# Own tile for M6+M1, tokens one pair ahead, late part splits, double raw weights, and a DVE swap in each pair of a fused channel-attention and FFN kernel

## The chip, the cores and the metric

The kernel runs on one core of one Trainium2 chip. The metric is device time in microseconds (us). The kernel before took 1188.86 us, the median of 3 runs (1186.72 to 1191.2). The profiled execution took 1185.15 us, of which its span, from the first to the last instruction, is 1183.3 us.

## What is computed

Channel attention over two batches of 6016 tokens and 256 channels, and on its result a feed-forward block with 2048 hidden units:

```python
qn = q / (norm(q, axis=1) + 1e-6);  kn = k / (norm(k, axis=1) + 1e-6)
s = softmax(kn.transpose(0, 2, 1) @ qn / tau)      # 256 x 256 per batch
x = (v @ s).reshape(12032, 256)
h = x @ w_in                                       # 256 -> 2048
g = h * (1 / (1 + exp(-h)))
out = g @ w_out                                    # 2048 -> 256
```

## The kernel before, in words

**Attention, 0 to about 98 us.** q and k stream in, TensorE sums the scores, DVE and ACT make norms and softmax. The softmax is folded into w_in (`fold`), so that v is never multiplied by it: each batch gets its own first weights. For the second batch they are saved to DRAM (`a1_dram`) and loaded again pair by pair (`load_a1`, `prepare_a1`, `split_a1`).

**Feed-forward, 98 us to the end.** 12 steps of tokens (`it` 0 to 11); a step holds two column halves of 512 tokens, steps 5 and 11 of 448. Each step runs over 8 pairs of hidden blocks; `n` = 8 * `it` + `pair` counts them through, 0 to 95. Both matrix products use a seven-product (Strassen-Winograd) scheme on 2x2 blocks; every product is three matmuls, since each operand is split into a rounded part and the rest (hi and lo): hi*hi, hi*lo, lo*hi. A pair from n = 9 on is 14 products, 42 matmuls: p1 to p7 of the first product (`product`, L802 to L804), and f22, f11, f21, f_t1 to f_t4 of the second (`second`, L860 to L862). Step 0 uses plain products for the second part (`output`, L847 to L851), 45 matmuls a pair.

**The engines' parts in a pair.** ACT copies the first product's sums out of PSUM (`seed_u1`, L1143, is its first on a new pair, then `copy_u`, `silu_c11`, `copy_w`), applies silu, rounds (`round_h`, `round_t13`, `round_t4`, `round_t2`) and flushes the product f21 to `fl` (`flush`). DVE makes C22 and C21 (`make_c22`, L1532, for which p4 waits; `make_c21`), the sums t1 to t4, and every "lo" part (`split_h`, L1546, and others). Each engine runs its list in order; nothing is reordered.

**Outputs.** The products M1, M3 to M7 gather in PSUM over the 8 pairs of a step. In the next step they are copied out: pair 0 `copy_m3`, `copy_m1` (to `o1`); pair 1 `copy_m7`, `copy_m4`, `copy_m5`; pair 2 `sum_u` on DVE (L1606) adds M6 to `o1` **in place**; pair 3 `make_nv`; pair 4 `sum_c22`. The output blocks are summed in DRAM by accumulating DMAs that POOL issues in order: `add_flushed` once a pair (`fl`, L627/L629), `add_o7` and `add_o1` in pair 1 (L640, L634), `add_u` in pair 2, `add_nv` in pair 3. `flush` of a pair waits until the `fl` store of the pair before has landed. `sum_u` writes the tile that `add_o1` reads, so it waits for that DMA's landing:

```python
dve.wait_ge(used_t2, PAIRS * it)
dve.wait_ge(o1_stored, 16 * it)
nc.vector.tensor_tensor(o1[:, 0:tok], m6[:, 0:tok], o1[:, 0:tok], ALU.add).then_inc(u_summed, 1)
```

`add_o7` stands ahead of `add_o1` on POOL and waits for `begin_c21`, an SP store that waits for `copy_m4` in pair 1.

**Tokens.** For the step to come, SP loads six blocks (`load_x`, in pair 7 before `load_ring_b`), POOL adds five more onto them by accumulating DMAs (`add_x_first`, three, in pair 2; `add_x_second` in pair 3; `add_x_third` in pair 6, after the split of T2), ACT rounds seven blocks in pairs 2 to 7 (`ROUND_X`) and DVE splits them in pairs 3 to 7 (`SPLIT_X`), T3 and T4 in the pair that rounds them.

**Second weights.** w_out's combinations for the later steps (8 parts) are made in steps 0 and 1: `load_part` on SP, `part` on POOL, `split_part` on DVE, `store_part` on SP; they come back each pair as `ring` (`load_ring_a`, 640 KB; `load_ring_b`, 256 KB).

## Time and profile before

| | before |
|---|---|
| median of 3 runs | 1188.86 us |
| profiled execution / its span | 1185.15 / 1183.3 us |
| TensorE busy with matmuls | 1065.1 us, 90% |
| DVE busy | 930.7 us, 79% |
| ACT busy | 912.0 us, 77% |
| POOL busy | 293.5 us, 25% |
| DMA queue of POOL (software) / of SP | 24.2% / 38.9% of 16 engines' span |
| mean granted TensorE clock | 0.963 |

Busy time of TensorE counts pipelined matmuls, so 90% doesn't mean that it runs at its peak 90% of the time. No engine is near 100%; what sets the time is read stage by stage from the waits and the timeline.

### The profile page before, as it was taken

The numbers are of one execution on the slowest core, as the hardware profiler recorded it, in microseconds if no ns is written. First come the engines' busy times: TensorE is split into PE (matmuls) and PEld (weight loads), VectorE is DVE, ScalarE is ACT, GpSimd is POOL, SyncE is SP. The second block draws the span as 40 slices with busy tenths as digits, with TensorE's granted clock in tenths as the row PEclk, the third lists the DMA queues.
The fourth block names the chain that finished last, engine by engine and source line by source line (L and its number), as shares of the span: only waits on it lengthen the run. The fifth ranks groups of instructions, "written<-read, shape, count | busy, mean of one in ns | idle before, by whom it ended". The sixth has DMA issues, their size and how long they took to land.

```text
span 1183.3 us, 15134 instructions
## 1 busy us (share of the span) xinstructions
PE 1065.1 (90%) x4584; PEld 862.6 (73%) x4584; DVE 930.7 (79%) x1306; ACT 912.0 (77%) x1581; POOL 293.5 (25%) x321
## 2 busy tenths in 40 slices
PE   9999899799899899899698898899799899899897
PEld 7987677577677677687587676687687687687786
DVE  6887665698698698698598898788688688688697
ACT  7988566687788788788577786788787788788775
POOL 3790430231211211211544351120211211211100
PEclk9999899999899899899899999999999999999899
DMA  9960722676676766666585774775675675674642
...
DMA packets 107841, 197.06 MB, mean 167 GB/s; under 512 B 9424, under 2 KB 42320, under 8 KB 107632
## 3 DMA queue, kind: packets, MB, share of 16 engines
q1 hardware_dynamic: 82720, 150.07, 38.9%
q0 software_dynamic: 24608, 45.39, 24.2%
...
q10 hardware_dynamic: 432, 0.62, 0.1%
...
## 4 chain that ended last, share of the span: by engine, by line
PE 50%; ACT 15%; DMA 13%; DVE 10%; issue 8%; SPq 1%; POOL 1%; DVEq 0%; ACTq 0%; POOLq 0%
PE ps_h L802 9%; DMA out_t_dram<-o_sb 8%; PE ps_h L803 8%; PE ps_h L804 8%; PE ps_o L860 5%; PE ps_o L861 5%; PE ps_o L862 5%; PE ps_h L860 3%; PE ps_h L862 3%; PE ps_h L861 3%; ACT ps_h L1043 3%; ACT gx_hi L1203 2%; ACT h L1159 2%; DVE g_lo L1546 2%; ACT w L1151 2%
## 5 line engine op out<-in xcount | busy, mean ns | idle before, releaser
L1546 DVE TENSOR_TENSOR g_lo<-h,g_hi 128x512 fp32r<-128x512 f32 (+1 forms) x296 | 204.0, 692 | 39.2 <-ACT g_hi L1182 36.6
L802 PE MATMUL ps_h<-b_hi,a_hi_mid 128*128 128x512 f32 (+1 forms) x336 | 141.4, 421 | 60.2 <-ACT h L1159 53.2
L627 POOL DMA_DIRECT2D out_t_dram<-fl_sb x70 | 60.6, 866 | 532.2 <-ACT fl_sb L1210 525.5
L1182 ACT ACTIVATE g_hi<-h 128x512 fp32r<-128x512 f32 (+1 forms) x296 | 182.5, 620 | 10.5 <-PE ps_h L862 3.8
L803 PE MATMUL ps_h<-b_lo,a_hi_mid 128*128 128x512 f32 (+1 forms) x336 | 136.0, 405 | 0.0
L804 PE MATMUL ps_h<-b_hi,a_lo_mid 128*128 128x512 f32 (+1 forms) x336 | 135.3, 403 | 0.0
L802 PEld LDWEIGHTS ps_h<-b_hi,a_hi_mid 128*128 128x128 f32 x336 | 67.1, 200 | 90.5 <-ACT h L1159 58.9
L860 PE MATMUL ps_h<-g_hi,ring 128*128 128x512 f32 (+1 forms) x264 | 103.6, 393 | 13.3 <-DVE h L1541 6.1
L1580 DVE TENSOR_TENSOR gx_lo<-t_raw,gx_hi 128x1024 fp32r<-128x1024 f32 (+1 forms) x88 | 107.0, 1216 | 1.0 <-ACT gx_hi L1189 0.9
L1558 DVE TENSOR_TENSOR t_raw<-h 128x1024 f32<-128x1024 f32 (+1 forms) x88 | 105.3, 1196 | 0.0
L860 PE MATMUL ps_o<-gx_hi,ring 128*128 128x512 f32 (+1 forms) x264 | 102.7, 389 | 0.7 <-DVE gx_lo L1590 0.4
L862 PE MATMUL ps_h<-g_hi,ring 128*128 128x512 f32 (+1 forms) x264 | 102.9, 390 | 0.0
L861 PE MATMUL ps_h<-g_lo,ring 128*128 128x512 f32 (+1 forms) x264 | 102.7, 389 | 0.0
L861 PE MATMUL ps_o<-gx_lo,ring 128*128 128x512 f32 (+1 forms) x264 | 102.4, 388 | 0.0
L862 PE MATMUL ps_o<-gx_hi,ring 128*128 128x512 f32 (+1 forms) x264 | 102.4, 388 | 0.0
L1203 ACT ACTIVATE gx_hi<-h 128x512 fp32r<-128x512 f32 (+1 forms) x88 | 54.3, 617 | 58.5 <-DVE h L1575 58.2
L1585 DVE TENSOR_TENSOR g_lo<-t_raw,g_hi 128x512 fp32r<-128x512 f32 (+1 forms) x88 | 60.8, 690 | 41.7 <-ACT g_hi L1197 41.2
L1189 ACT ACTIVATE gx_hi<-t_raw 128x1024 fp32r<-128x1024 f32 (+1 forms) x88 | 90.5, 1028 | 0.8 <-PE ps_o L862 0.7
L1210 ACT ACTIVATE fl_sb<-ps_h 128x512 f32<-128x512 f32 (+1 forms) x81 | 48.0, 593 | 54.9 <-PE ps_h L862 53.7
L1172 ACT ACTIVATE h<-h 128x512 f32<-128x512 f32 (+1 forms) x96 | 59.5, 620 | 38.6 <-DVE h L1532 38.0
L802 PE MATMUL ps_h<-b_hi,a_hi_last 128*128 128x512 f32 (+1 forms) x168 | 67.4, 401 | 23.4 <-DVE h L1532 23.4
L1541 DVE TENSOR_TENSOR h<-ps_h,u 128x512 f32<-128x512 f32 (+1 forms) x96 | 65.1, 678 | 22.4 <-PE ps_h L804 21.8
...
## 6 DMA issues: line engine op xcount, KB each, us to landing
ring<-s_dram SPq DMA_DIRECT2D x88, 640.0 KB, 4.9
ring<-s_dram SPq DMA_DIRECT2D x88, 256.0 KB, 3.2
out_t_dram<-fl_sb POOLq DMA_DIRECT2D x72, 256.0 KB, 5.8
x_raw<-v_t_dram SPq DMA_DIRECT2D x58, 256.0 KB, 4.0
x_raw<-v_t_dram POOLq DMA_DIRECT2D x45, 256.0 KB, 6.5
out_t_dram<-o_sb POOLq DMA_DIRECT2D x36, 256.0 KB, 5.2
out_t_dram<-o_sb SPq DMA_DIRECT2D x27, 256.0 KB, 2.7
...
```

The lines of the kernel that those rows point to most:

```text
L802: nc.tensor.matmul(out, w_hi, x_hi, start=start, stop=False, skip_group_check=True)
L803: nc.tensor.matmul(out, w_hi, x_lo, start=False, stop=False, skip_group_check=True)
L804: return nc.tensor.matmul(out, w_lo, x_hi, start=False, stop=True, skip_group_check=True)
L860: nc.tensor.matmul(out[:, 0:tok], w_hi, x_hi[:, 0:tok], start=start, stop=False, skip_group_check=True)
L861: nc.tensor.matmul(out[:, 0:tok], w_hi, x_lo[:, 0:tok], start=False, stop=False, skip_group_check=True)
L862: return nc.tensor.matmul(out[:, 0:tok], w_lo, x_hi[:, 0:tok], start=False, stop=True, skip_group_check=True)
L1182: nc.scalar.activation(g_hi[:, g, 0:tok], h[:, g, 0:tok], ACT.Copy).then_inc(hi[g], 1)
L1189: nc.scalar.activation(gx_hi[:, GT1:GT3 + 1, 0:tok], t13_raw[:, :, 0:tok], ACT.Copy).then_inc(t13_hi, 1)
L1203: nc.scalar.activation(gx_hi[:, GT4, 0:tok], h[:, H21, 0:tok], ACT.Copy).then_inc(t4_hi, 1)
L1546: nc.vector.tensor_tensor(g_lo[:, g, 0:tok], h[:, g, 0:tok], g_hi[:, g, 0:tok].bitcast(F32), ALU.subtract).then_inc(lo[g], 1)
L1558: nc.vector.tensor_tensor(t13_raw[:, :, 0:tok], h[:, H11:H12 + 1, 0:tok], h[:, H12:H22 + 1, 0:tok], ALU.add).then_inc(t13_made, 1)
L1580: nc.vector.tensor_tensor(gx_lo[:, GT1:GT3 + 1, 0:tok], t13_raw[:, :, 0:tok], gx_hi[:, GT1:GT3 + 1, 0:tok].bitcast(F32), ALU.subtract).the ...
```

## The change

- `sum_u` writes a tile of its own, `u_sum`; its wait for `add_o1`'s landing becomes one for the copy of M1, and for the output work of the step before. `copy_m1` now waits for the landing of `add_o1` of the step before.
- Tokens: `add_x_first`, `add_x_second`, `add_x_third` go from pairs 2, 3, 6 to 0, 1, 5 (from step 2 on; for step 2's tokens the old places stay). ACT's roundings are reordered, one pair ahead of DVE's splits. TensorE's p4 alone waits for the last group. `load_x` goes behind `load_ring_b` and `load_a1`.
- Raw second-batch weights and their sums get two tiles each, with new places of the reload.
- DVE: `make_c22` goes ahead of `split_h(H11)` in each pair. In step 0 the part and token splits go to the end of a pair, one part a pair from pair 1; `split_part` of the turning pair (n = 8) goes to its end; `sum_c22` from pair 4 to 5.
- POOL rounds three quarters of w_out instead of ACT; SP's `load_x(1)` goes ahead of the wait for the folds; ACT loads the silu table early; the last C12 store goes from POOL to ACT.

```diff
+        u_sum = sb("u_sum_sb", [P, TOK])
+        a1_raw1 = sb("a1_raw1", [P, 4, P])
+        sums1 = sb("sums1", [P, 4, P])
...
-        reload_at = {SWITCH + max(2 * pair - 1, 0): pair for pair in range(PAIRS)}
+        reload_at = {SWITCH + 1 + 3 * pair // 2 + pair // 6: pair for pair in range(PAIRS)}
...
             def load_a1(pair):
                 sp.wait_ge(a_split, PAIRS)
-                if pair:
-                    sp.wait_ge(a1_split, pair)
-                sp.dma_start(a1_raw[:], a1_dram[:, pair]).then_inc(a1_loaded, 16)
+                if pair >= 2:
+                    sp.wait_ge(a1_split, pair - 1)
+                sp.dma_start(a1_raw[pair % 2][:], a1_dram[:, pair]).then_inc(a1_loaded[pair % 2], 16)
...
+            sp.wait_ge(v_split, 3)
+            load_x(1)
             sp.wait_ge(wp_summed, 2 * FOLDS)
             load_part(0)
             load_part(1)
-            sp.wait_ge(v_split, 3)
-            load_x(1)
...
-                if pair == PAIRS - 1 and it + 2 < ALL:
-                    sp.wait_ge(x_split, 3 + FACTORS * it)
-                    load_x(it + 2)
                 load_ring_b(n)
                 if n + 1 in reload_at:
                     load_a1(reload_at[n + 1])
+                if pair == PAIRS - 1 and it + 2 < ALL:
+                    sp.wait_ge(x_split, x_groups(it + 1))
+                    load_x(it + 2)
...
+            for n in range(1, PARTS):
+                round_wo(n)
             add_x_first(1)
             part(0)
...
-                if pair == 2 and it + 1 < ALL:
+                if pair == (0 if it > 1 else 2) and it + 1 < ALL:
                     add_x_first(it + 1)
-                if pair == 3 and it + 1 < ALL:
+                if pair == (1 if it > 1 else 3) and it + 1 < ALL:
                     add_x_second(it + 1)
-                if pair == 6 and it + 1 < ALL:
+                if pair == (5 if it > 1 else 6) and it + 1 < ALL:
                     add_x_third(it + 1)
...
                 if it > 1:
-                    act.wait_ge(c21_stored, 32 * (it - 1))
+                    act.wait_ge(o1_stored, 16 * (it - 1))
+                    act.wait_ge(u_summed, it - 1)
                 nc.scalar.activation(o1[:, 0:tok], m1[:, 0:tok], ACT.Copy).then_inc(o1_copied, 1)
...
-            ROUND_X = {2: (B11, B21), 3: (B22,), 4: (T2,), 5: (T1,), 6: (T3,), 7: (T4,)}
+            ROUND_X_SECOND = {2: (B11, B21), 3: (B22,), 4: (T2, T1), 5: (T3,), 7: (T4,)}
+            ROUND_X = {2: (B11, B21), 3: (T2, B22), 4: (T1,), 5: (T3,), 6: (T4,)}
...
-            SPLIT_X_FIRST = {4: (T1, T3), 5: (B11, B22), 7: (T4, T4)}
-            SPLIT_X = {3: (B11,), 4: (B21,), 5: (B22, T2), 6: (T1, T3), 7: (T4,)}
+            SPLIT_X_FIRST = {3: (T1, T2), 4: (T3, T3), 6: (B11, B22), 7: (T4, T4)}
+            SPLIT_X_SECOND = {3: (B11, B21), 4: (B22,), 5: (T2, T1), 6: (T3,)}
+            SPLIT_X = {3: (B11,), 4: (B21, T2), 5: (B22,), 6: (T1, T3), 7: (T4,)}
...
                 dve.wait_ge(used_t2, PAIRS * it)
-                dve.wait_ge(o1_stored, 16 * it)
-                nc.vector.tensor_tensor(o1[:, 0:tok], m6[:, 0:tok], o1[:, 0:tok], ALU.add).then_inc(u_summed, 1)
+                dve.wait_ge(o1_copied, it)
+                if it > 1:
+                    dve.wait_ge(c21_stored, 32 * (it - 1))
+                    dve.wait_ge(nv_made, it - 1)
+                nc.vector.tensor_tensor(u_sum[:, 0:tok], m6[:, 0:tok], o1[:, 0:tok], ALU.add).then_inc(u_summed, 1)
...
-            PARTS_AT = {2: (0, 1), 3: (2,), 4: (3,), 6: (4,), 8: (5,), 10: (6,), 12: (7,)}
+            PARTS_AT = {1: 0, 2: 1, 3: 2, 4: 3, 6: 4, 8: 5, 10: 6, 12: 7}
...
+                if PAIRS - EARLY - 1 <= n < PAIRS - 1:
+                    split_a(0, n + 1)
+                if n < PAIRS - 2:
+                    sum_a(0, n + 2)
+                if n in PARTS_AT:
+                    split_part(PARTS_AT[n])
                 if n in SPLIT_X_FIRST:
                     split_x(1, *SPLIT_X_FIRST[n])
...
+                make_c22(n, tok)
                 split_h(n, tok, H11)
-                make_c22(n, tok)
                 split_t2(n - 1, before)
```

## Rows read from the trace of the kernel before

**Rows 1.** Waits, whole run: who waited for whom: us in total, times, longest

```profile
DVE o_sb L1606 <- DMA out_t_dram<-o_sb: 58.9, 10, 10.1
PEld ps_h L802 <- DVE h L1532: 47.1, 49, 2.2
DVE b_lo L1507 <- ACT b_hi L1129: 22.4, 20, 1.5
```

**Rows 2.** Timeline, ACT's L1143 at seven pair starts: start us, us, instruction

```profile
117.48 0.60 ACT L1143 ACTIVATE ps_h<-ps_h 128x512 f32<-128x512 f32 x1
201.68 0.58 ACT L1143 ACTIVATE ps_h<-ps_h 128x512 f32<-128x512 f32 x1
292.76 0.59 ACT L1143 ACTIVATE ps_h<-ps_h 128x512 f32<-128x512 f32 x1
302.37 0.59 ACT L1143 ACTIVATE ps_h<-ps_h 128x512 f32<-128x512 f32 x1
...
557.34 0.54 ACT L1143 ACTIVATE ps_h<-ps_h 128x448 f32<-128x448 f32 x1
741.07 0.59 ACT L1143 ACTIVATE ps_h<-ps_h 128x512 f32<-128x512 f32 x1
1093.05 0.54 ACT L1143 ACTIVATE ps_h<-ps_h 128x448 f32<-128x448 f32 x1
```

**Rows 3.** Timeline, step 2, pair 2; in brackets idle before and releaser

```profile
310.68 1.22 POOL L634 DMA_DIRECT2D out_t_dram<-o_sb  x1
311.98 0.57 POOL L629 DMA_DIRECT2D out_t_dram<-fl_sb  x1
319.01 0.69 DVE L1606 TENSOR_TENSOR o_sb<-ps_o,o_sb 128x512 f32<-128x512 f32 x1 [6.08 <-DMA out_t_dram<-o_sb]
321.50 0.79 PE L802 MATMUL ps_h<-b_hi,a_hi_mid 128*128 128x512 f32 x1 [5.70 <-ACT h L1159]
```

**Rows 4.** Windows: stretch, length; busy (instructions) by engine; granted clock, DMA share, GB/s

```profile
322.00:325.00 3.00, 3.00 (x8) 2.31 (x7) 1.42 (x3) 2.11 (x5) 1.53 (x2) 0.51 1.02 155
347.40:357.50 10.10, 9.89 (x44) 7.80 (x43) 9.31 (x14) 8.72 (x15) 0.87 (x1) 1.00 0.48 117
357.50:368.50 11.00, 9.83 (x43) 7.77 (x42) 9.34 (x14) 8.72 (x15) 1.76 (x2) 1.00 0.62 135
```

**Rows 5.** Timeline, step 2, pair 6, around C22

```profile
363.72 0.69 DVE L1507 TENSOR_TENSOR b_lo<-x_raw,b_hi 128x512 fp32r<-128x512 f32 x1 [0.86 <-ACT b_hi L1129]
...
365.67 0.50 PE L802 MATMUL ps_h<-b_hi,a_hi_last 128*128 128x512 f32 x1 [1.17 <-DVE h L1532]
```

**Rows 6.** DMA issues, 309 to 322 us: KB each, us to landing

```profile
ring<-s_dram SPq DMA_DIRECT2D x1, 640.0 KB, 9.2
out_t_dram<-fl_sb POOLq DMA_DIRECT2D x1, 256.0 KB, 8.1
```

**Rows 7.** Timeline, steps 5 and 6, the reload: ring wait, output wait, preparation's ends

```profile
580.35 0.47 PE L860 MATMUL ps_h<-g_hi,ring 128*128 128x448 f32 x1 [4.21 <-DMA ring<-s_dram]
587.66 0.69 DVE L1606 TENSOR_TENSOR o_sb<-ps_o,o_sb 128x512 f32<-128x512 f32 x1 [10.11 <-DMA out_t_dram<-o_sb]
...
601.12 2.12 POOL L664 TENSOR_TENSOR sums<-a_raw 128x128 f32<-128x128 f32 x1
607.38 1.01 POOL L675 CAST a_hi_mid<-sums 128x512 fp32r<-128x512 f32 x1
```

**Rows 8.** Timeline, step 0: the tokens of step 1, and TensorE's longest stop

```profile
125.83 2.80 POOL L582 DMA_DIRECT2D x_raw<-v_t_dram  x3 [35.83 <-DMA x_raw<-v_t_dram]
...
142.64 0.79 PE L847 MATMUL ps_o<-g_hi,wo_hi 128*128 128x512 f32 x1 [4.78 <-DVE g_lo L1546]
```

**Rows 9.** Timeline, attention: a POOL cast alone, a DVE sum beside a POOL instruction

```profile
45.43 1.04 POOL L535 CAST w_in_hi<-w_in_raw 128x1024 fp32r<-128x1024 f32 x1
...
84.95 2.82 DVE L1433 TENSOR_TENSOR square_sum<-square_sum 128x512 f32<-128x512 f32 x1
```

**Rows 10.** Timeline, step 1, pair 2: ACT waits for the tokens

```profile
232.68 1.15 ACT L1129 ACTIVATE b_hi<-x_raw 128x512 fp32r<-128x512 f32 x2 [6.45 <-DMA x_raw<-v_t_dram]
```

More of the change, by code:

```diff
@@ L277, in channel_attention_ffn @@
         used_t4 = sem("used_t4")
-        part_loaded = sem("part_loaded")
+        part_loaded = [sem(f"part_loaded{n}") for n in range(2)]
         part_step = sem("part_step")
@@ L285, in channel_attention_ffn @@
         a1_saved = sem("a1_saved")
-        a1_loaded = sem("a1_loaded")
+        a1_loaded = [sem(f"a1_loaded{n}") for n in range(2)]
         a1_step = sem("a1_step")
@@ L345, in width, with x_groups, x_place @@
             return tokens_of(n // PAIRS)[1]
-        reload_at = {SWITCH + max(2 * pair - 1, 0): pair for pair in range(PAIRS)}
+        reload_at = {SWITCH + 1 + 3 * pair // 2 + pair // 6: pair for pair in range(PAIRS)}
+        assert all(SWITCH + pair < n <= SWITCH + PAIRS - 2 + pair for n, pair in reload_at.items())
+        X_FIRST = ((T1, T2), (T3, T3), (B11, B22), (T4, T4))
+        X_SECOND = (B11, B21, B22, T2, T1, T3, T4)
+        X_LATER = (B11, B21, T2, B22, T1, T3, T4)
+        def x_groups(step):
+            return len(X_FIRST) + FACTORS * (step - 1)
+        def x_place(step, block_):
+            if step == 1:
+                return 1 + [block_ in range(a, b + 1) for a, b in X_FIRST].index(True)
+            return x_groups(step - 1) + 1 + (X_SECOND if step == 2 else X_LATER).index(block_)
         def part_tiles(i):
@@ L493, in _ @@
                     begin_c21(it - 1)
-                if it > 1 and pair == 4:
+                if it > 1 and pair == 5:
                     store_c22(it - 1)
-                if pair == PAIRS - 1 and it + 2 < ALL:
-                    sp.wait_ge(x_split, 3 + FACTORS * it)
-                    load_x(it + 2)
                 load_ring_b(n)
@@ L596, in add_x_third @@
             def add_x_third(step):
-                if step == 1:
-                    pool.wait_ge(x_split, 1)
-                else:
-                    pool.wait_ge(x_split, 3 + FACTORS * (step - 2) + 4)
+                pool.wait_ge(x_split, x_place(step, T2))
                 add_x(step, X_T2, 1, 0).then_inc(t_third, 16)
@@ L655, in prepare_a1 @@
             def prepare_a1(pair):
-                a12, a22, a11, a21 = (a1_raw[:, j, :] for j in range(4))
-                s1, s2, s3, s4 = (sums[:, j, :] for j in range(4))
-                pool.wait_ge(a1_loaded, 16 * (pair + 1))
-                if pair:
-                    pool.wait_ge(a1_split, pair)
+                raw, totals = a1_raw[pair % 2], a1_sums[pair % 2]
+                a12, a22, a11, a21 = (raw[:, j, :] for j in range(4))
+                s1, s2, s3, s4 = (totals[:, j, :] for j in range(4))
+                pool.wait_ge(a1_loaded[pair % 2], 16 * (pair // 2 + 1))
+                if pair >= 2:
+                    pool.wait_ge(a1_split, pair - 1)
                 else:
@@ L673, in prepare_a1 @@
                 pool.wait_ge(p4_done, SWITCH + pair + 1)
-                nc.gpsimd.tensor_copy(a_hi(pair)[:, 0:3, :], a1_raw[:, 0:3, :])
-                nc.gpsimd.tensor_copy(a_hi(pair)[:, 3:7, :], sums[:]).then_inc(a1_rounded, 1)
+                nc.gpsimd.tensor_copy(a_hi(pair)[:, 0:3, :], raw[:, 0:3, :])
+                nc.gpsimd.tensor_copy(a_hi(pair)[:, 3:7, :], totals[:]).then_inc(a1_rounded, 1)
             split_rows(0)
@@ L834, in p4 @@
                 pe.wait_ge(c22_made, n + 1)
+                if pair == 0 and n:
+                    pe.wait_ge(x_split, x_groups(n // PAIRS))
                 product(pair, par, tok, BANK_Y, A22, T4, False).then_inc(p4_done, 1)
@@ L1259, in opening_pair @@
                 seed_u1(0, TOK)
-                round_wo(1)
+                nc.scalar.activation(scratch[:, 0:1], ones[:, 0:1], ACT.Silu)
                 copy_folded(1, 0)
@@ L1296, in first_step @@
                 copy_w(n, TOK)
+                if n >= 3 and n - 3 < len(X_FIRST):
+                    round_x(1, *X_FIRST[n - 3])
                 silu_c22(n, TOK)
@@ L1344, in pair_step @@
                 if it < FINAL:
-                    for block_ in ROUND_X.get(pair, ()):
+                    for block_ in (ROUND_X if it > 1 else ROUND_X_SECOND).get(pair, ()):
                         round_x(it + 1, block_, block_)
@@ L1667, in pair_step @@
                     make_nv(it - 1)
-                if it > 1 and pair == 4:
+                if it > 1 and pair == 5:
                     sum_c22(it - 1)
@@ L1673, in pair_step @@
                 if it < FINAL:
-                    for block_ in SPLIT_X.get(pair, ()):
+                    for block_ in (SPLIT_X if it > 1 else SPLIT_X_SECOND).get(pair, ()):
                         split_x(it + 1, block_, block_)
+                make_c22(n, tok)
                 split_h(n, tok, H11)
-                make_c22(n, tok)
                 split_t2(n - 1, before)
                 make_c21(n, tok)
-                for i in PARTS_AT.get(n, ()):
-                    split_part(i)
+                if it == 1 and pair == PAIRS - 1:
+                    split_x(2, T4, T4)
+                if n in PARTS_AT:
+                    split_part(PARTS_AT[n])
                 if n - 1 in reload_at:
```

89 lines of the change are left out of this document (42 added, 47 removed).

## The prediction, made before the changed kernel was run

> **What bounds the kernel now.** I read four views in this order. First the waits of the whole run, to see which long waits are on an engine that the others need. DVE waits ten times, once for each output step, 58.9 us in all, for a DMA to land before `sum_u` [rows 1]; TensorE waits 49 times for C22, and DVE 20 times for a rounded token block [rows 1]. POOL's far longer waits don't count: POOL is idle three quarters of the time. Second the starts of the pairs, by ACT's first copy of a pair. The pair from 292.76 to 302.37 us took 9.61 us [rows 2] for its 42 matmuls, 0.229 us each: that is TensorE without a stop, the floor of a wide pair, and 8 of them make 76.9 us. But steps 2 to 4 took 557.34 - 292.76 = 264.6 us and steps 7 to 10 took 1093.05 - 741.07 = 352.0 us [rows 2]: seven wide steps, 616.6 us, 88.1 each. So 11.2 us of each step is lost. Third the timeline of one step, to see where. In pair 2 DVE stands 6.08 us before `sum_u`, everything behind it in DVE's list stands too, and TensorE stands 5.70 us [rows 3]. After that the granted clock is 0.51, the 1.2 GHz level, and 8 matmuls take 3.00 us [rows 4], which is 0.375 us each or more; some 9 matmuls at about 0.2 us too much are 1.8 us. In pairs 6 and 7 DVE waits 0.86 us for ACT's rounding, then splits the block, then H11, and only then makes C22; TensorE stands 1.17 us, and the granted clock stays 1.00 (2.4 GHz) [rows 4, 5]. Two of those with their restart are 2.8 us. 5.7 + 1.8 + 2.8 = 10.3 of the 11.2; the other 0.9 us are C22 waits of 0.1 to 0.4 us in the pairs between. Fourth the DMA views, for what comes next (below).
>
> **The wait for `add_o1` goes.** `sum_u` keeps its place, but its last wait is now a copy of pair 0. Its other new waits are on output work of the step before, over 60 us old. Nobody else waits for the landing until `copy_m1` of the next step, 80 us later. The addition costs DVE 0.69 us [rows 3], as `make_nv` does in pair 3, which has no stop of its own. Gain 5.7 + 1.8 = 7.5 us a step. The gain of the clock rests on there being no other long stop: the 1.17 us ones don't lower it [rows 4, 5].
>
> **C22 ahead of H11, roundings a pair ahead.** C22 needs p7 and `copy_w`, which are done when the second token split ends in a pair with two. Without the 0.86 us wait and without the 0.6 us of H11 in front of it [rows 5], C22 comes 1.4 to 1.5 us earlier, which is more than 1.17 us. H11's lo part is wanted only in the next pair. In pairs without a token block C22 now waits for p7 with H11 behind it, and C21 behind both; but C21 needs p4, nine matmuls (2.1 us) after p7, and C22, H11 and T2, some 0.6 us from start to start, take 1.9 us of that. Close, but it fits. Gain 2.8 + most of 0.9, I take 3.2 us a step (bounds 2.4 and 3.7).
>
> **What is late next: POOL's DMA queue.** `flush` of pair 3 needs the landing of pair 2's `fl` store. That store is issued right behind `add_o1`, at 311.98, and takes 8.1 us [rows 3, 6]: it lands at 320.1. With no stop, pair 3 begins 9.61 us after pair 2 and ACT wants the landing at about 320.7; only 0.6 us are left, and there is no slack between flush, seed and p6. The ring's 640 KB, issued at the same time, took 9.2 us [rows 6] and are wanted at about 322. The change puts `add_x_second` in front of that store. Its price: pair 6 has one accumulate of this kind more than pair 5, and the DMA engines' busy time is 0.62 x 11.0 = 6.8 against 0.48 x 10.1 = 4.8 us [rows 4], so 2.0 us if nothing overlaps, and nothing if it does. A few microseconds later in this pair the DMA engines are fully busy (share 1.02) [rows 4]. I take 1.4 us later, so a stop of 0.8 us in each step; bounds 0 and 3 (the whole 2.0 and a crowded pair 1: three `add_x_first`, 6 us of engine time, now fall in pair 0 beside the six loads). The three were behind `add_u` in pair 2 before and leave it. Wide step after: 76.9 + 0.5 (left-over C22 waits) + 0.8 = 78.2; seven steps 547.4; **gain 69.2 us** (bounds 77 and 50).
>
> **Reload, steps 5 and 6.** They took 741.07 - 557.34 = 183.7 us [rows 2] where the pairs' floors are 8 x 8.6 (448 tokens) + 76.9 = 145.7. With one raw tile, `load_a1` waits for the split of the pair before, and SP's ring load and `begin_c21` stand behind it: TensorE waits 4.21 us for the ring, DVE 10.11 us for `add_o1` [rows 7]. Two tiles take that away. What stays: each of 8 `split_a1` adds about 1.15 us to a DVE list that is busy 9.3 us in a pair with two token splits [rows 4], about 0.8 us over the floor, 6 us in all. New: `prepare_a1` takes POOL 7.3 us beside a busy DVE, from 601.12 to 608.39 [rows 7]. It now stands in pairs 1 and 2 of step 5, between the output DMAs and the `fl` store. The store of pair 2 then goes out about 9 us into the pair instead of 1, lands some 3 us after `flush` wants it, and the next is again about 2 us late: 5 us. Together with 5 us of DVE slowed beside POOL (it was so before): 145.7 + 16.3 = 162.0, **gain 21.7 us** (bounds 28 and 12).
>
> **Step 11** has the `sum_u` wait, no token blocks: **gain 7 us**.
>
> **Step 0.** POOL waits for the token loads at 125.83, then makes the parts; DVE's part splits wait for them in pair 2, and TensorE stands 4.78 us behind DVE [rows 8], with the slow clock after. Now the tokens come while SP idles, the part splits stand at the end of a pair, where DVE otherwise waits about 3 us for p7. Pairs 1 to 7 took 201.68 - 117.48 = 84.2 us [rows 2]; the floor is 45 x 0.229 = 10.3 each. I take 10.5, plus 1.15 us each in front of pairs 6 and 7, where `split_a` (a_lo wanted by p1) now stands behind H12: 75.8, gain 8.4. Three w_out roundings leave ACT in pair 0; TensorE is nearly without a stop there: gain 1.0. They go to POOL, 1.04 us each [rows 9], 3.1 us from 90.0 on, beside the DVE chain of the second softmax, for which TensorE waits. A DVE sum took 2.82 us beside a POOL instruction, 0.7 alone [rows 9]; the chain's instructions there mostly read PSUM or one operand; bounds 0 and 2.1, I take 0.5. **Gain 8.9 us** (bounds 11 and 3).
>
> The Trainium skill (SBUF — State Buffer, Who interferes with whom) says that a DVE instruction with two SBUF inputs contends with a GpSimd instruction that reads SBUF, and that one with at most one such input does not. That speaks against this move only if POOL's casts reach the chain's one multiplication of two SBUF tiles, at 93.55 us; the 2.82 us row agrees with the rule, and by it the cost would be 0, or at most one cast, 1.04 us.
>
> **Step 1** took 292.76 - 201.68 = 91.1 us. Its 6.45 us wait for tokens [rows 10] is not touched: `load_x(2)` still stands on SP behind the store of part 5, and that part's split, now at the end of the turning pair, is 1.7 us later. C22 and the roundings give about 4.5 in pairs 4 to 7. **Gain 3 us** (bounds 6 and -2). The last store's move to ACT is off the last chain: 0.
>
> **Sum.** 69.2 + 21.7 + 7 + 8.9 + 3 = 109.8 us. 1185.15 - 109.8 = 1075.4 us for an execution like the profiled one; the median of the runs is 3.7 us above it, so **1079 us**.
>
> **Rivals.** *The queue takes the place of the wait.* For it: 0.6 us of slack, DMA engines fully busy for a time in this pair [rows 4]. Against it: `fl`'s store landed only 1.2 us behind `add_o1` (318.9 and 320.1), so DMAs in this queue overlap. If `add_x_second` costs its whole latency like `add_o1` did, 5 to 6 us, pair 3 stops 4.4 us, the clock falls again, 6.3 us instead of 0.8 in ten steps: 1079 + 55 = 1134 us. Chance 0.11. The Trainium skill (DMA: Bandwidth & Descriptors, Queues, rings and completion order) says that a completion count is written only behind every earlier write of the same DMA engine, across its queues. By that `fl` can't be told as landed before the token block in front of it; how much that is it doesn't say, and it would give a time between the two.
>
> *POOL's DMAs are served one by one and become the bound; the kernel is slower.* 17 a step (8 `fl`, 4 outputs, 5 tokens). At 5.2 us each in order a step would be 88 us as before, and above that every step is slower: at 5.5 us 93.5, some 5.4 more in ten steps, +54, less 12 from steps 0 and 1: about 1230 us. The overlap of 1.2 us speaks against it: it decides only if tokens and stores packed into pairs 0 and 1 lose that overlap. Chance 0.02.
>
> *The stop stays*, since `sum_u` is not what TensorE needs: only the other terms, 109.8 - 10 x 7.5 = 35: 1144 us. The 5.70 us on TensorE right behind the 6.08 on DVE speaks against it. Chance 0.02.
>
> *Better than forecast*: no queue stop, POOL out of the way in step 5: about 1060 and below. Chance 0.05.
>
> **How the numbers follow.** The forecast has 0.80. Its own bounds, added as if independent around 1079, give about 1062 to 1105; the range goes a little towards the queue rival: 1060 to 1112. A measurement of this kernel tells about 0.5%, 6 us, from no change. All cases but one are far beyond that on the fast side: faster 0.97, slower 0.02, within 0.5% 0.01.
>
> **What would show it.** No idle time of DVE before `sum_u`; the store of `u_sum` issued 3 us into pair 2 instead of 9; no granted clock near 0.5 in steps 2 to 4; no wait of `b_lo` for `b_hi`; 78 us from step to step; a wait of ACT's `flush` for the landing of `fl` at pair 3 of about 0.8 us, and of 2 to 3 us at pairs 3 and 4 of step 5. The forecast is wrong if `flush` or the ring waits over 3 us in the common steps, or if DVE, with 9.3 us of work in a pair of 9.6 [rows 4], is late for other reasons than DMAs: then TensorE waits for C21, T4 or H11 where nothing does today.

## The result, and the profile after

The changed kernel takes **1072.47 us** (median of 4 runs, 1070.89 to 1073.94) against 1188.24 us (4 runs, 1186.72 to 1191.2): a ratio of 0.9023, 95% interval 0.9000 to 0.9046. The forecast was 1079 us. The profiled execution took 1070.89 us, its span 1069.1 us.

The page after, busy times and two rows of the 40 slices:

```profile
PE 1034.2 (97%) x4584; PEld 851.6 (80%) x4584; DVE 934.1 (87%) x1307; ACT 898.7 (84%) x1580; POOL 297.6 (28%) x323
...
PE   9999998989999999999978999999999999999997
...
PEclk9999999999999999999999999999999999999999
```

TensorE is now busy 97% of the span, and none of the 40 slices has a mean granted clock under 0.9; shorter drops are left (last section). The waits of the whole run that answer to [rows 1] (who waited for whom: us in total, times, longest):

```profile
DVE h L1558 <- PE ps_h L825: 41.7, 46, 5.2
...
ACT fl_sb L1234 <- DMA out_t_dram<-fl_sb: 9.5, 9, 2.8
...
PEld ps_h L823 <- DVE h L1558: 5.8, 9, 1.6
```

DVE's 58.9 us of waiting for `add_o1` have no row any more, nor have its waits for a rounded token block. TensorE's weight loads waited 47.1 us in 49 waits for C22 and wait 5.8 us in 9; it is DVE that now waits for TensorE before it can make C22, 41.7 us in all. The starts of pairs after, answering to [rows 2] (timeline, ACT's first copy: steps 0, 1, 2, its second and third pair, steps 5, 7 and 11):

```profile
99.76 0.61 ACT L1167 ACTIVATE ps_h<-ps_h 128x512 f32<-128x512 f32 x1
195.41 0.58 ACT L1167 ACTIVATE ps_h<-ps_h 128x512 f32<-128x512 f32 x1
280.54 0.59 ACT L1167 ACTIVATE ps_h<-ps_h 128x512 f32<-128x512 f32 x1
290.18 0.59 ACT L1167 ACTIVATE ps_h<-ps_h 128x512 f32<-128x512 f32 x1
300.76 0.59 ACT L1167 ACTIVATE ps_h<-ps_h 128x512 f32<-128x512 f32 x1
...
512.38 0.54 ACT L1167 ACTIVATE ps_h<-ps_h 128x448 f32<-128x448 f32 x1
679.80 0.59 ACT L1167 ACTIVATE ps_h<-ps_h 128x512 f32<-128x512 f32 x1
987.93 0.54 ACT L1167 ACTIVATE ps_h<-ps_h 128x448 f32<-128x448 f32 x1
```

Differences of these rows and of the rows of before give the account by part, in us:

| part | before | after | gain | forecast gain (bounds) |
|---|---|---|---|---|
| to the first pair | 100.9 | 99.8 | 1.2 | with step 0 |
| step 0 | 100.7 | 95.6 | 5.1, 6.3 with the opening | 8.9 (3 to 11) |
| step 1 | 91.1 | 85.1 | 5.9 | 3 (-2 to 6) |
| steps 2 to 4, 7 to 10 | 616.6 | 540.0 | 76.6 | 69.2 (50 to 77) |
| steps 5 and 6 | 183.7 | 167.4 | 16.3 | 21.7 (12 to 28) |
| step 11 and the end | 90.3 | 81.2 | 9.1 | 7 |
| span | 1183.3 | 1069.1 | 114.2 | 109.8 |

Windows of two plain steps (8 and 9) and of the reload steps (5 and 6) after, columns as in [rows 4]:

```profile
512.38:679.80 167.42, 153.09 (x674) 124.94 (x673) 157.88 (x212) 134.36 (x250) 78.02 (x99) 0.99 0.73 180
756.86:911.08 154.22, 154.22 (x674) 125.92 (x673) 141.24 (x196) 138.65 (x250) 29.10 (x35) 1.00 0.75 184
```

In plain steps TensorE is busy all of the 154.22 us, at a granted clock of 1.00 (2.4 GHz). Two floors of 76.9 us are 153.8 us, so at most some 0.4 us are left to gain there outside TensorE. DVE is busy 92% of that time.

### The profile page after: what moved, and what is told of

The parts are those of the page before. It is cut to its first block, busy times and chain, and to the rows that moved or that the text cites. A ratio compares the mean times of both kernels' runs of the same rounds, so it can differ in the third digit from the quotient of the medians.

```text
span 1069.1 us, 15160 instructions
## 1 busy us (share of the span) xinstructions
PE 1034.2 (97%) x4584; PEld 851.6 (80%) x4584; DVE 934.1 (87%) x1307; ACT 898.7 (84%) x1580; POOL 297.6 (28%) x323
## 4 chain that ended last, share of the span: by engine, by line
PE 71%; DVE 6%; ACT 3%; issue 3%; DMA 2%; SPq 1%; DVEq 0%; POOL 0%; ACTq 0%; POOLq 0%
PE ps_h L823 12%; PE ps_h L825 12%; PE ps_h L824 12%; PE ps_o L883 6%; PE ps_o L884 6%; PE ps_o L885 6%; PE ps_h L883 5%; PE ps_h L885 5%; PE ps_h L884 5%; DVE t_raw L1584 1%; DVE g_lo L1572 1%; DMA ring<-s_dram 1%; PE ps_o L870 1%; PE ps_o L872 1%; PE ps_o L874 1%
## 5 line engine op out<-in xcount | busy, mean ns | idle before, releaser
L1206 ACT ACTIVATE g_hi<-h 128x512 fp32r<-128x512 f32 (+1 forms) x296 | 182.5, 620 | 10.2 <-PE ps_h L885 3.8
L823 PE MATMUL ps_h<-b_hi,a_hi_mid 128*128 128x512 f32 (+1 forms) x336 | 132.7, 395 | 6.1 <-ACT h L1183 3.1
L825 PE MATMUL ps_h<-b_hi,a_lo_mid 128*128 128x512 f32 (+1 forms) x336 | 130.9, 390 | 0.0
L824 PE MATMUL ps_h<-b_lo,a_hi_mid 128*128 128x512 f32 (+1 forms) x336 | 130.7, 389 | 0.0
L1558 DVE TENSOR_TENSOR h<-ps_h,w 128x512 f32<-128x512 f32 (+1 forms) x96 | 65.2, 679 | 61.5 <-PE ps_h L825 41.7
L883 PE MATMUL ps_h<-g_hi,ring 128*128 128x512 f32 (+1 forms) x264 | 103.7, 393 | 13.5 <-DVE g_lo L1572 7.2
L823 PEld LDWEIGHTS ps_h<-b_hi,a_hi_mid 128*128 128x128 f32 x336 | 63.5, 189 | 27.3 <-ACT h L1183 5.5
L1171 ACT ACTIVATE u<-ps_h 128x512 f32<-128x512 f32 (+1 forms) x96 | 56.7, 590 | 23.8 <-PE ps_h L825 21.4
L1449 DVE TENSOR_TENSOR square_sum<-ps_h,square_sum 128x768 f32<-128x768 f32 (+2 forms) x66 | 57.5, 912 | 18.3 <-ACT ps_h L1067 17.1
L825 PEld LDWEIGHTS ps_h<-b_hi,a_lo_mid 128*128 128x128 f32 x336 | 63.6, 189 | 12.4
L883 PEld LDWEIGHTS ps_h<-g_hi,ring 128*128 128x128 f32 x264 | 49.9, 189 | 29.3 <-issue 13.7
```

The lines of the kernel that those rows point to most:

```text
L823: nc.tensor.matmul(out, w_hi, x_hi, start=start, stop=False, skip_group_check=True)
L824: nc.tensor.matmul(out, w_hi, x_lo, start=False, stop=False, skip_group_check=True)
L825: return nc.tensor.matmul(out, w_lo, x_hi, start=False, stop=True, skip_group_check=True)
L883: nc.tensor.matmul(out[:, 0:tok], w_hi, x_hi[:, 0:tok], start=start, stop=False, skip_group_check=True)
L1206: nc.scalar.activation(g_hi[:, g, 0:tok], h[:, g, 0:tok], ACT.Copy).then_inc(hi[g], 1)
L1558: nc.vector.tensor_tensor(h[:, H22, 0:tok], ps_h[:, BANK_Y, 0:tok], w[:, 0:tok], ALU.add).then_inc(c22_made, 1)
```

## The experiments

All times are medians of the runs of each kernel; all are to be read against 1072.47 and, for the kernel before run beside them, 1188 to 1189 us. Times of steps and pairs are those of one profiled execution each. In plain steps they mostly agree within 0.6 us where nothing was edited, but step 5 does not repeat so well: it took 84.2 us after and 88.5 us in a kernel in which nothing of it was edited, and 86.7 and 81.9 us in two kernels whose code for it is the same. A difference of under 5 us in step 5 therefore shows little by itself.

**Is it the wait of `sum_u`?** One kernel puts the sum back into M1's tile, one adds only the new tile to the kernel before.

```diff
...
-                nc.vector.tensor_tensor(u_sum[:, 0:tok], m6[:, 0:tok], o1[:, 0:tok], ALU.add).then_inc(u_summed, 1)
+                dve.wait_ge(o1_stored, 16 * it)
+                nc.vector.tensor_tensor(o1[:, 0:tok], m6[:, 0:tok], o1[:, 0:tok], ALU.add).then_inc(u_summed, 1)
...
```

> The kernel after, with one part undone: M6+M1 is summed in the tile of M1 again, so VectorE's sum waits until the accumulating DMA has read that tile; all the rest (swaps, tokens a pair ahead, the rotated parts and raw weights) stays. Theory A (the prediction's first step): that wait alone is worth 5.7 us of stop and about 1.8 us of slow clock in each of some ten steps, so the time is 1072 + 75 = about 1147 us, and pair 2 of a wide step is back near 17 us from 9.9. Theory B (the wait was only the last of several things late in that pair, and the swaps and the earlier roundings removed most of it on their own): 1085 to 1100 us, with pair 2 at 11 to 12 us.

Measured 1147.88 us (1144.85 to 1148.27). The stop is back in its old place; timeline of step 3, pair 2 (DVE's sum, TensorE's next product):

```profile
394.42 0.69 DVE L1630 TENSOR_TENSOR o_sb<-ps_o,o_sb 128x512 f32<-128x512 f32 x1 [6.23 <-DMA out_t_dram<-o_sb]
...
396.91 0.80 PE L823 MATMUL ps_h<-b_hi,a_hi_mid 128*128 128x512 f32 x1 [5.79 <-ACT h L1183]
```

Theory A holds to 1 us: 75.4 us for ten waits. The parts are less even than the sum: a plain step takes 85.2 us for 77.0, step 11 7.1 us more, and steps 5 and 6 only 11.4 us more together.

> The kernel before with only the tile of its own for M6+M1 added. Theory A (the parts add up, each in its own place): it gains the same 75 us, to about 1113 us; pair 2 of a wide step falls from 17.3 to about 9.9 us and pairs 6 and 7 stay at 11.1 us, since their stops belong to the order of VectorE's work. Theory B (the parts need one another: the accumulating DMAs, the roundings or the loads of tokens move up and stop the next pair once the wait is gone): 1130 to 1150 us, with new stops in pairs 3 to 5.

Measured 1121.01 us (1116.55 to 1123.77): a gain of 67.8, not 75, and between the two theories. Plain steps fell from 88.1 to 80.5 us. But step 8 took 84.8 us, with this wait in its pair 3, theory B in one step:

```profile
833.00 0.60 ACT L1211 ACTIVATE fl_sb<-ps_h 128x512 f32<-128x512 f32 x1 [3.55 <-DMA out_t_dram<-fl_sb]
```

And steps 5 and 6 gained only 5.1 us together; TensorE still waits 4.65 us for the ring there, as in [rows 7], a wait that is gone after. The parts add up almost: 67.8 for the tile alone and 41.0 for all the rest (1188.84 - 1147.88) are 108.8 of 116.

**The two edits of pairs 6 and 7.** Undone singly and together:

```diff
+                split_h(n, tok, H11)
                 make_c22(n, tok)
-                split_h(n, tok, H11)
```

```diff
-            ROUND_X = {2: (B11, B21), 3: (T2, B22), 4: (T1,), 5: (T3,), 6: (T4,)}
+            ROUND_X = {2: (B11, B21), 3: (T2, B22), 4: (T1,), 6: (T3,), 7: (T4,)}
```

> The kernel after, with the split of H11 ahead of C22 again in each pair. Theory A (the swap and the earlier roundings must both be there: either alone still leaves the pairs with two token splits late): C22 then lies behind H11's split, but the roundings that the splits wait for come a pair earlier than before; the lateness falls from 1.17 us to some 0.3 to 0.5 us in two pairs of ten steps, and TensorE loses nearly no clock: 1072 + 8 = about 1080 us. Theory B (the swap does the whole work): the stops of 1.17 us with their slow clock come back, 2 x 1.4 x 8 to 10 steps: 1094 to 1100 us. Theory C (the swap does nothing): 1072 us.

> The kernel after, with the last two token roundings (T3, T4) a pair later again, as before the change; the swap stays. Theory A (both edits share the gain of pairs 6 and 7): the splits wait for the rounding behind ScalarE's queue, some 0.5 us in each of the two pairs: 1072 + 11 = about 1083 us. Theory B (the rounding's place was the whole stop): 2 x 1.4 us x 8 to 10 steps more, 1094 to 1100 us. Theory C (its place does nothing once C22 is ahead): 1072 us.

> The kernel after, with both edits of VectorE's last two pairs undone together: H11 is split ahead of C22 again, and the roundings of T3 and T4 are a pair later. Undone singly they cost 16.2 us (the swap: 1088.65) and 17.7 us (the roundings: 1090.21), against 1072.47. Theory A (the two are links of one chain, whose lateness each shortens by a part): together they cost what the prediction took for the pair of them or a bit more, 10 steps x 2 pairs x 1.4 us = 28 to 34 us, so 1100 to 1107 us, with pairs 6 and 7 of a wide step at 11.1 us from 9.6. Theory B (either alone is enough to bring the whole stop back, so both together cost no more than one): about 1090 us.

Measured 1088.65 us (1084.34 to 1096.67), 1090.21 us (1085.19 to 1093.60) and 1107.95 us (1105.39 to 1109.87). Waits in steps 3 and 4 without the swap:

```profile
PEld ps_h L823 <- DVE h L1558: 3.3, 8, 0.7
```

with the late roundings:

```profile
DVE b_lo L1533 <- ACT b_hi L1153: 4.6, 4, 1.5
...
PEld ps_h L823 <- DVE h L1558: 3.8, 4, 1.0
```

and with both undone:

```profile
PEld ps_h L823 <- DVE h L1558: 7.8, 9, 1.6
PE ps_h L823 <- DVE h L1558: 4.6, 5, 1.2
DVE b_lo L1533 <- ACT b_hi L1153: 4.6, 4, 1.5
```

Without the swap, pairs 4 and 6 took 10.1 us; with the late roundings pairs 6 and 7 took 10.45; with both undone pairs 6 and 7 took 11.1, as before the change. The plain steps (3, 4, 7 to 10) took 77.0 us after, 78.0, 78.6 and 80.5 us in these three. The two single times lie between theories A and B; that with both undone is 1 us above theory A's range and far from B's 1090. So the part of theory A that holds is the mechanism: one chain, which each edit shortens. In a plain step the two together (3.4 us) are worth more than the sum of the two taken singly (1.0 + 1.6), which fits a slack of DVE that the first lateness uses up; over the whole kernel 35.5 us stand against 16.2 + 17.7. 80.5 is also what the kernel with only the new tile has, so these two edits account for all of the rest of a plain step. My sizes for the single ones were too low, 8 and 11 for 16 and 18 us. I had given each of ten steps the same small loss. The profiled execution without the swap stood 13.5 us above that after; 7.1 of them were in the seven plain wide steps, near what I had said for those, but 5.4 in the reload and 2.8 in step 1 (step 0 gave 1.5 back).

**How near is the DMA queue?**

```diff
+                if it > 1 and pair == 1:
+                    more = ones[:].rearrange("p (one f) -> p one f", one=1).to_broadcast([P, 4, P])
...
+                        nc.gpsimd.dma_start(extra_dram, more, accum_op=ALU.add).then_inc(extra_stored, 16)
```

> The kernel after, with one more accumulating DMA of 256 KB in each wide step, issued by GpSimd in pair 1 ahead of the store of the folded product: a constant tile is added into a tensor in DRAM that nothing reads. It asks how much slack the order of these DMAs has before they stop TensorE again. Theory A (the queue has slack: the sum of M6+M1 that the step needs no longer waits for it, only ScalarE's writers of the folded tiles do, some 0.2 us a step): one more transfer of 2 to 3 us in the queue moves those landings by as much; below 10 steps x 2 us = 20 us, I expect 5 to 15 us, 1077 to 1087 us. Theory B (the queue is the next bound, so each transfer added shows whole, with the slow clock behind it): 10 x (2.5 + 1) = 35 us, about 1107 us. Theory C (nothing waits): 1072 us.

Measured 1094.72 us (1089.39 to 1097.25), +22, between A and B: the slack is used up. DMA issues of the `fl` store of pair 2, step 3 (KB each, us to landing), after:

```profile
x_raw<-v_t_dram POOLq DMA_DIRECT2D x1, 256.0 KB, 7.3
out_t_dram<-fl_sb POOLq DMA_DIRECT2D x1, 256.0 KB, 7.5
```

and with the extra transfer:

```profile
extra_dram<-ones POOLq DMA_DIRECT2D x1, 256.0 KB, 8.9
out_t_dram<-fl_sb POOLq DMA_DIRECT2D x1, 256.0 KB, 9.2
```

The timeline of that pair with the extra transfer, and the window behind the stop:

```profile
389.73 0.60 ACT L1244 ACTIVATE fl_sb<-ps_h 128x512 f32<-128x512 f32 x1 [3.04 <-DMA out_t_dram<-fl_sb]
...
391.39 0.50 PE L833 MATMUL ps_h<-b_hi,a_hi_mid 128*128 128x512 f32 x1 [2.23 <-ACT ps_h L1177]
```

```profile
391.40:394.40 3.00, 3.00 (x13) 2.50 (x14) 3.00 (x5) 2.88 (x5) 0.93 (x2) 1.00 0.95 122
```

ACT's wait before `flush` is 3.04 us where it is 0.83 after: 2.2 us more. Of the 3.04 us, 2.23 reach TensorE. The clock stays 1.00 behind this stop, so the 10 us that theory B gave to the clock don't come. The order of the DMAs in pairs 1 and 2 is at its limit: 256 KB more in each of ten steps cost 22 us, 2.2 us each.

**What keeps the reload steps long?** Pairs of the reload moved, GpSimd's work on A1 left out, and that work in four instructions.

```diff
-        reload_at = {SWITCH + 1 + 3 * pair // 2 + pair // 6: pair for pair in range(PAIRS)}
+        reload_at = {SWITCH + at: pair for pair, at in enumerate((3, 4, 6, 7, 8, 11, 12, 13))}
```

> The kernel after, with the eight reloads of A1 in the sixth and seventh steps placed at other pairs (offsets 3, 4, 6, 7, 8, 11, 12, 13 behind the first half's last pair, in place of 1, 2, 4, 5, 7, 8, 11, 12), so that GpSimd's four sums and two roundings of A1 stay off the pairs in which VectorE has the largest token split. Steps 5 and 6 took 167.4 us against 154.2 for two steps without a reload. Theory A (VectorE late by its own and GpSimd's work in one pair): some 5 us of these 13 come back, about 1067 us. Theory B (each reload costs its time wherever it stands): 1072 us within 2.

Measured 1068.42 us (1067.59 to 1071.84), ratio interval 0.8986 to 0.9025, which overlaps that of after. In the profiled execution steps 5 and 6 took 167.7 us: 3.3 us less in step 5, 3.6 more in step 6. Given how step 5 scatters, that shows no gain in these steps and no loss: theory B as far as can be told; a gain of some us elsewhere is neither shown nor excluded.

```diff
-                nc.gpsimd.tensor_tensor(s1, a22, a21, ALU.subtract).then_inc(a1_step, 1)
...
-                nc.gpsimd.tensor_copy(a_hi(pair)[:, 0:3, :], raw[:, 0:3, :])
-                nc.gpsimd.tensor_copy(a_hi(pair)[:, 3:7, :], totals[:]).then_inc(a1_rounded, 1)
+                nc.gpsimd.tensor_copy(a_hi(pair)[:, 0:1, 0:2], raw[:, 0:1, 0:2]).then_inc(a1_rounded, 1)
...
```

DVE's split of the sums reads the raw blocks there instead, in the same shape.

> The kernel after, with GpSimd's work on the reloaded A1 left out: the sums of its blocks and the roundings into the high halves are not made (one rounding of two columns stays for the order), so the second half's products use old values. ScalarE's and VectorE's work on A1 and the DMAs stay. Theory A (GpSimd beside VectorE slows VectorE's operations in the reload steps, up to 3 us for one of them): of the 13.2 us that steps 5 and 6 stand above two plain steps 7 to 10 go, so 1063 to 1066 us, and the operations of 2.8 to 3.1 us in those steps are gone. Theory B (the stops there are VectorE's own added splits of A1 and the store of the folded product): at most 2 us go, 1070 to 1072 us.

Measured 1057.77 us (1057.12 to 1058.1): -14.7, more than theory A gave. The window of steps 5 and 6 without GpSimd's work:

```profile
510.98:664.09 153.11, 148.28 (x674) 124.22 (x673) 140.89 (x212) 132.67 (x250) 32.01 (x43) 1.00 0.79 197
```

GpSimd is busy 46 us less, DVE 17.0 us less for the same 212 instructions, and the two steps are 14.3 us shorter, far more than step 5 scatters. (The expectation set the surplus of these steps at 13.2 us over two plain ones; step 5 is narrower, so against the floors of 145.7 us it was 21.7.) Which DVE instructions were slowed is seen by form (busy us, mean ns; group by line and shape), after:

```profile
L1584 DVE TENSOR_TENSOR t_raw<-h 128x896 f32<-128x896 f32 x8 | 10.7, 1336 | 0.0
...
L1601 DVE TENSOR_TENSOR h<-t_raw,h 128x448 f32<-128x448 f32 x8 | 7.3, 909 | 0.5
...
L1567 DVE TENSOR_TENSOR h<-ps_h,u 128x448 f32<-128x448 f32 x8 | 4.9, 614 | 0.0
```

and without GpSimd's work, the same three (L1574, L1591, L1557 there):

```profile
L1574 DVE TENSOR_TENSOR t_raw<-h 128x896 f32<-128x896 f32 x8 | 8.7, 1082 | 0.0
...
L1591 DVE TENSOR_TENSOR h<-t_raw,h 128x448 f32<-128x448 f32 x8 | 5.0, 623 | 0.5
...
L1557 DVE TENSOR_TENSOR h<-ps_h,u 128x448 f32<-128x448 f32 x8 | 5.0, 619 | 0.0
```

The two forms with two SBUF inputs took 23% and 46% longer in the mean, the one with an input from PSUM no longer at all. The Trainium skill (SBUF — State Buffer, Who interferes with whom) says that a DVE instruction with two SBUF inputs contends with a GpSimd instruction that reads SBUF, and that one with at most one SBUF input, outside DVE's 2-port perf modes, does not. For these forms this trace agrees. GpSimd's work also stands in front of output stores on its queue, so the 14.3 us hold both the slower DVE and any store that went out late; how `flush` waited without that work is told below.

```diff
-                nc.gpsimd.tensor_tensor(s1, a22, a21, ALU.subtract).then_inc(a1_step, 1)
...
+                nc.gpsimd.tensor_tensor(totals[:, 0:3:2, :], raw[:, 1:3, :], raw[:, 3:4, :].to_broadcast([P, 2, P]),
+                                        ALU.subtract).then_inc(a1_step, 1)
...
+                nc.gpsimd.tensor_tensor(s2, s1, a11, ALU.add).then_inc(a1_step, 1)
...
+                nc.gpsimd.tensor_tensor(s4, s2, a12, ALU.subtract).then_inc(a1_step, 1)
...
+                nc.gpsimd.tensor_scalar(s2, s2, -1.0, None, ALU.mult).then_inc(a1_step, 1)
```

> The kernel after, with GpSimd's sums of each reloaded pair of A1 made by four instructions over five blocks (one subtraction over two blocks, an addition, a subtraction and a multiplication by -1) in place of six over six; the values are the same. Without all of GpSimd's work on A1, VectorE's busy time in steps 5 and 6 fell from 157.9 to 140.9 us, GpSimd's from 78.0 to 32.0, the two steps from 167.4 to 153.1 us and the kernel by 14.7 us: 0.37 us of VectorE and 0.31 us of the span per us of GpSimd. Theory A (VectorE is slowed in proportion to GpSimd's element work beside it): two of six sums of some 1.06 us each are saved in eight pairs, 46 us falls to 29 to 33 us, and 4 to 5 us of the span go: about 1068 us. Theory B (GpSimd's time is by elements and the wider subtraction takes twice one, so only one sixth of the sums goes): 8 x 1.06 = 8.5 us of GpSimd, 2.6 us of the span: about 1070 us. Theory C (the roundings into the high halves do the harm, not the sums): 1072 us.

Measured 1069.57 us (1069.03 to 1075.63), ratio interval 0.8988 to 0.9037, no difference that can be told. The window of steps 5 and 6:

```profile
513.30:684.56 171.26, 154.31 (x674) 125.91 (x673) 156.77 (x212) 134.59 (x249) 69.35 (x83) 0.98 0.72 176
```

GpSimd is 8.7 us less busy, as theory B had said (8.5), so theory A falls. But DVE is only 1.1 us less busy, not the 3 us that 0.37 us per us of GpSimd would give, and the kernel of the three edits below, with the same four sums, has the same 1.1 (156.81 against 157.88 us). GpSimd's busy time is no measure of what DVE loses. This execution was the slowest of the five, and its two steps took 3.8 us more than those after, so it shows no gain of the span. Whether the elements that GpSimd reads set DVE's loss, or the roundings more than the sums (theory C), stays open.

**Step 0 and step 1.**

```diff
                 make_c22(n, TOK)
+                if PAIRS - EARLY - 1 <= n < PAIRS - 1:
+                    split_a(0, n + 1)
...
                 split_h(n, TOK, H12)
-                if PAIRS - EARLY - 1 <= n < PAIRS - 1:
-                    split_a(0, n + 1)
```

> The kernel after, with the two splits of A for pairs 6 and 7 (first step, pairs 5 and 6) placed right behind C22, where VectorE stands idle for 1.8 us, in place of behind H12's split. In the profile after, the two stops of TensorE for M1 are 2.10 and 1.49 us and these pairs take 12.85 and 12.92 us (12.0 to 13.6 in the other kernels). Theory A (VectorE is late by the split's own time): both stops shrink by most of 1.2 us each, pairs 5 and 6 take 11.4 to 11.9 us, and 2 to 3.5 us of the time go: 1069 to 1070.5 us. Theory B (the split waits for the roundings of A on ScalarE, wherever it stands): 1072 us within 1.

Measured 1072.15 us (1068.82 to 1073.79), as after. Yet theory A was right for the two pairs. After, the two products waited for the split (timeline):

```profile
170.20 0.75 PE L823 MATMUL ps_h<-b_hi,a_hi_last 128*128 128x512 f32 x1 [2.10 <-DVE a_lo_last L1519]
...
183.77 0.50 PE L823 MATMUL ps_h<-b_hi,a_hi_last 128*128 128x512 f32 x1 [1.49 <-DVE a_lo_last L1519]
```

Moved, both stops are gone, pairs 5 and 6 take 10.2 and 10.3 us (12.9 and 12.9 after), and step 0 gains 5.6 us. Of these 3.3 are lost again right behind: step 1 takes 88.4 us against 85.1, 2.1 of them in its pair 2, by this wait:

```profile
220.99 1.15 ACT L1153 ACTIVATE b_hi<-x_raw 128x512 fp32r<-128x512 f32 x2 [5.54 <-DMA x_raw<-v_t_dram]
```

It was 3.65 us after. The token loads stand on SP behind the landing of part 5's store and of the outputs that share `x_raw`. SP issued them 5.5 us earlier than after (211.70 for 217.24 us), nearly as much as the pair moved (5.9), but ACT had the tokens only 4.0 us earlier; what held the loads back is not shown. Step 2 took 1.3 us more and step 5 4.3, with 12.1 to 13.0 us in its pairs 2 to 5, and nothing of them was edited; why stays open.

> The kernel after, with three edits together: the splits of A behind C22 in pairs 5 and 6 of the first step, the four sums in place of six on GpSimd for each reloaded pair, and, on SyncE in the second step, the stores of the scaled outputs issued ahead of its wait for the stored part, so that the load of the ring's next weights does not queue behind them (TensorE's stop of 3.4 us in pair 2 of that step). If each does what it does alone and they don't touch one another: 2 to 3.5 + 3 to 5 + 0 to 3 us, so about 1064 us (1061 to 1068). If the stop of the second step is set by GpSimd's DMAs and not by SyncE's order, its pair 2 stays at 14 us and the sum is 5 to 8 us: 1065 to 1067 us.

The third of these edits, in SP's list:

```diff
+            store_std_outputs()
             sp.wait_ge(part_stored, part_stored_by(5))
             load_part(6)
-            store_std_outputs()
```

Measured **1066.35 us** (1064.14 to 1068.88), ratio 0.8976 (0.8954 to 0.8998), just below that of after: faster than both kernels. Step 0 keeps its 5.6 us (90.0), and with the outputs stored first step 1 takes 84.8 us, its pair 2 12.3 and not 14:

```profile
218.08 1.15 ACT L1153 ACTIVATE b_hi<-x_raw 128x512 fp32r<-128x512 f32 x2 [2.23 <-DMA x_raw<-v_t_dram]
```

Alone, neither the splits nor the four sums gave a difference that can be told, and the order of the stores was not tried alone, so what each of the three gives is not separated.

> The kernel of the three edits, with the eight reloads of A1 moved to the other pairs as well (offsets 3, 4, 6, 7, 8, 11, 12, 13). Moved alone, they gave 1068.42 us against 1072.47, but in the profiled execution steps 5 and 6 took 167.7 us, no less than 167.4. Theory A (each reload costs its time wherever it stands, as the profiled execution says): the same as the kernel of the three edits within 1 us. Theory B (the 4 us were real, and outside of these two steps): 3 to 4 us less than it.

Measured 1064.76 us (1064.26 to 1071.05), ratio 0.8977 (0.8953 to 0.9000): no difference from the kernel of the three edits that can be told. Theory A; between these two placements of the reload no difference is shown.

## Why the prediction was right, step by step

- **The wait for `add_o1` goes.** Right. Forecast 7.5 us a step, 75 in ten; put back it costs 75.4 us, and 8.2 us in a plain step (85.2 against 77.0). That the total is right to 1 us is partly luck: the plain steps were dearer than 7.5, the reload steps cheaper (11.4 for two).
- **C22 ahead of H11, roundings a pair ahead.** Right, slightly low: forecast 3.2 us a step (2.4 to 3.7), measured 3.4. That both are needed together, which the prediction said only by adding 0.86 and 0.6 us, is shown by the three kernels.
- **What is late next: the queue.** The place was right, the size too large. Timeline of step 3, pair 2 to 3, after:

```profile
383.78 0.85 POOL L667 DMA_DIRECT2D out_t_dram<-u_sum_sb  x1 [3.21 <-DMA out_t_dram<-o_sb]
386.55 0.60 ACT L1234 ACTIVATE fl_sb<-ps_h 128x512 f32<-128x512 f32 x1 [0.83 <-DMA out_t_dram<-fl_sb]
```

  The store of `u_sum` went out 6.2 us into pair 2, not 3 as I had said. It starts 3.21 us late for the landing of `add_o7`, and nobody waits for it. ACT waits 0.83 us as forecast (0.8), but the pairs around it, 9.94 and 9.47 us, are only 0.2 above two of 9.61: ACT's wait is not TensorE's stop. I had said that there is no slack between `flush`, seed and p6; some 0.6 us are there. That and left-over C22 waits of nearly nothing, not 0.5, are the 7.4 us by which seven wide steps beat the sum. The rival that the queue takes the wait's place is nearer than the result alone tells: one transfer more costs 2.2 us a step, though not the 5.5 us of the rival: the stop is shorter, and the clock stays.
- **Reload.** 16.3 us, forecast 21.7 (12 to 28); the term that was too small is, as far as the runs separate it, the 5 us for DVE beside GpSimd. The wait of `flush` at pair 3 of step 5 came as said; timeline:

```profile
538.88 0.60 POOL L650 DMA_DIRECT2D out_t_dram<-fl_sb  x1
...
540.31 3.12 DVE L1584 TENSOR_TENSOR t_raw<-h 128x896 f32<-128x896 f32 x1
...
542.00 0.54 ACT L1234 ACTIVATE fl_sb<-ps_h 128x448 f32<-128x448 f32 x1 [2.84 <-DMA out_t_dram<-fl_sb]
542.44 0.57 ACT L1206 ACTIVATE g_hi<-h 128x448 fp32r<-128x448 f32 x1
...
543.35 0.87 DVE L1572 TENSOR_TENSOR g_lo<-h,g_hi 128x448 fp32r<-128x448 f32 x1
...
544.37 0.44 PE L883 MATMUL ps_h<-g_hi,ring 128*128 128x448 f32 x1 [3.67 <-DVE g_lo L1572]
```

  The `fl` store stands behind `prepare_a1`, ACT waits 2.84 us (forecast 3), but the second wait, of about 2 us at pair 4, has no row; two smaller ones (1.18 and 0.61 us) stand ahead, at pairs 1 and 2. TensorE's 3.67 us end on DVE's `g_lo`, and two late things meet before it: DVE's sum, 3.12 us where its kind takes 1.08, ends at 543.43, and ACT's `g_hi`, which waited behind the late `flush`, at 543.01. Without the slow sum this stop would be only some 0.3 us shorter (an estimate from these rows), so the two terms that I had added overlap here. Waits of `flush` in steps 5 and 6, after and without GpSimd's work on A1:

```profile
ACT fl_sb L1234 <- DMA out_t_dram<-fl_sb: 4.6, 3, 2.8
...
ACT fl_sb L1224 <- DMA out_t_dram<-fl_sb: 3.8, 2, 2.0
```

  These waits are nearly the same without it, so `prepare_a1` in front of the store, which I had named as their cause, is not the main one. Of the 21.7 us over the floors, 14.3 go with GpSimd's work, where I had 5 us for DVE and 5 for the stores behind `prepare_a1`; 7.4 stay, where I had 6 for the splits. Since `flush` waits almost as long without that work, most of the 14.3 us is left to the slower DVE, but no run separates the two. I took those 5 as unchanged from before; but before, DVE was busy 152.9 of 183.7 us in these steps, and after 157.9 of 167.4, so that little idle time is left to cover what it loses. That the two raw tiles took the 4.21 us wait for the ring away was not tried by itself either; what is shown is that the wait stays with the new tile for `sum_u` alone.
- **Step 0.** 6.3 us with the opening, forecast 8.9 (3 to 11). The 1.0 that I took for pair 0 came as 0.4 (16.16 us for 16.55). The opening took 1.2 us less, where I had a loss of 0.5 for w_out's roundings on POOL; but with the same opening it took 98.5 to 100.1 us in the kernels of this case, and 99.6 with the old one, so neither a gain nor a loss is shown there. Pairs 1 to 7 took 79.5 us, not 75.8. Pair 4 took 1.1 us more than I had (11.6 us), which I did not follow up. The larger term that failed is `split_a` behind H12, 1.15 us each: the stops are 2.10 and 1.49 us, each pair is 2.5 above 10.3 or so, and the experiment gave 5.2 us back in these two pairs. The first split took 1.67 us (168.48 to 170.15), the second 1.16; that the products wait 0.3 to 0.4 us longer than that, and that a pair loses more than its stop, the sum had not. What adds it wasn't tried by itself.
- **Step 1.** 5.9 us, forecast 3. Its wait for tokens was not untouched, as I said, but fell from 6.45 us [rows 10] to 3.65. Why it did wasn't tried by itself; with other orders ahead of it the wait was 5.54 and 2.23 us.
- **Step 11**: 9.1 us, forecast 7. The wait was worth what I had: put back, it costs step 11 7.1 us. The rest is mostly the last C12 store, whose move from POOL to ACT I had put at nothing ("off the last chain"): from the issue of the very last store to the end of the span it is 4.16 us in both kernels that leave the C12 store on POOL (before, and the new tile alone), and 2.4 to 2.6 us in all twelve others. Nothing else was edited there, but the move was not undone by itself.
- **Rivals.** None took place. For the rival that the stop stays, the sum has a slip: 1079 + 75 is 1154 us, not 1144; its chance does not hang on that.
- **The number.** The errors of the parts, +7.4 and +2.9 and +2.1 against -5.4 and -2.6, cancel in part, and that is luck: the sum is 4.4 us off. Another 2.1 us are the step from the profiled execution to the median, taken as 3.7 us from before and 1.6 after. Together they are the 6.5 us between 1079 and 1072.47.
